# Up projection by seven half-size products for fourteen of twenty-four blocks, on one core

## The reference, cut to what matters

```python
def _moe2_ref(x, w_in, w_out, g_ln):          # x 3072 x 512, w_in 512 x 1024, w_out 1024 x 512
    h = x @ w_in
    e = np.exp(h - np.max(h, axis=-1, keepdims=True))
    solu = h * (e / (np.sum(e, axis=-1, keepdims=True) + 1e-09))
    mu = np.mean(solu, axis=-1, keepdims=True)
    var = np.mean((solu - mu) ** 2, axis=-1, keepdims=True)
    return ((solu - mu) / np.sqrt(var + 1e-06) * g_ln) @ w_out
```

## Time and profile before

| | us |
|---|---|
| three runs: median (lowest, highest) | 971.77 (971.66, 973.21) |
| the profiled execution | 974.78 |
| its span, first to last instruction | 972.9 |
| PE busy | 941.5 (97%) |
| DVE busy | 643.6 (66%) |
| ACT busy | 521.7 (54%) |
| POOL busy | 136.1 (14%) |

### The profile page before, as it was taken

The page is one execution under the profiler, slowest core; times in us unless marked ns, Lnnn a source line. Parts: engine busy times, 40 slices in busy tenths (PEclk is TensorE's granted clock), DMA queues, the critical chain, the costliest instruction groups (busy, mean ns, idle before and its releaser), DMA issues.

```text
span 972.9 us, 14652 instructions
## 1 busy us (share of the span) xinstructions
PE 941.5 (97%) x5334; PEld 832.9 (86%) x5334; DVE 643.6 (66%) x1065; ACT 521.7 (54%) x911; POOL 136.1 (14%) x170
## 2 busy tenths in 40 slices
PE   7979999999999999999999999999999999999996
PEld 4666787787799999999999999999988888888875
DVE  3767885786778755454568877777475775666641
ACT  3554654555555533342546554555477876666632
POOL 4313401101115330000044001010100000000000
PEclk9989999999999999999999999999999999999999
DMA  9746635626153413131374617250520154351533
GB/s 264 215 155 201 183 153 174 184 115 182 55 210 120 157 71 130 49 115 66 111 247 143 229 52 248 87 191 17 170 75 32 27 137 96 88 141 34 112 86 84
DMA packets 103847, 126.61 MB, mean 130 GB/s; under 512 B 8160, under 2 KB 84320, under 8 KB 103776
## 3 DMA queue, kind: packets, MB, share of 16 engines
q1 hardware_dynamic: 98320, 109.28, 36.6%
q0 software_dynamic: 4736, 15.73, 4.7%
q10 hardware_dynamic: 720, 0.66, 0.3%
HBM read 77.41 MB, written 37.75 MB: 118 GB/s over the span
## 4 chain that ended last, share of the span: by engine, by line
PE 79%; DVE 7%; DMA 4%; issue 3%; ACT 3%; SPq 2%; POOL 2%; DVEq 0%; ACTq 0%; POOLq 0%
PE psum L949 10%; PE psum L952 10%; PE psum L951 10%; PE psum L385 8%; PE psum L386 8%; PE psum L387 8%; PE psum L985 6%; PE psum L987 6%; PE psum L988 6%; PE psum L842 3%; PE psum L876 2%; PE psum L866 2%; PE psum L855 2%; DMA w_raw<-weights 1%; DMA v_buf<-v_rows 1%
## 5 line engine op out<-in xcount | busy, mean ns | idle before, releaser
L949 PE MATMUL psum<-xo_hi,w_hi 128*128 128x384 f32 x560 | 195.1, 348 | 7.8 <-DVE psum L1658 2.6
L951 PE MATMUL psum<-xo_lo,w_hi 128*128 128x384 f32 x560 | 188.3, 336 | 0.0
L952 PE MATMUL psum<-xo_hi,w_lo 128*128 128x384 f32 x560 | 188.1, 336 | 0.0
L949 PEld LDWEIGHTS psum<-xo_hi,w_hi 128*128 128x128 f32 x560 | 105.8, 189 | 13.9 <-DVE xo_lo L1644 4.1
L951 PEld LDWEIGHTS psum<-xo_lo,w_hi 128*128 128x128 f32 x560 | 105.9, 189 | 0.8 <-issue 0.3
L952 PEld LDWEIGHTS psum<-xo_hi,w_lo 128*128 128x128 f32 x560 | 105.8, 189 | 0.0
L1163 ACT ACTIVATE xo_hi<-b 128x768 fp32r<-128x768 f32 x84 | 70.6, 846 | 63.2 <-PE psum L988 49.5
L1538 DVE TENSOR_TENSOR xo_lo<-b,xo_hi 128x768 fp32r<-128x768 f32 x84 | 81.2, 969 | 34.5 <-ACT xo_hi L1163 34.3
L385 PE MATMUL psum<-w_out_hi,ln_t_hi 128*128 128x512 f32 x192 | 75.1, 391 | 2.1 <-DVE ln_t_lo L1775 2.1
L1658 DVE TENSOR_TENSOR psum<-psum,p_buf 128x384 f32<-128x384 f32 x48 | 27.1, 564 | 75.0 <-PE psum L952 75.0
L385 PE MATMUL psum<-w_in_hi,x_hi 128*128 128x512 f32 x192 | 75.3, 392 | 0.4 <-ACT h_buf L1284 0.4
(11 more groups left out here) (142 smaller groups left out, 2025.2 us busy)
## 6 DMA issues: line engine op xcount, KB each, us to landing
act_dram<-act_buf SPq DMA_DIRECT2D x48, 384.0 KB, 2.4
b<-act_dram SPq DMA_DIRECT2D x48, 384.0 KB, 4.9
ln_t<-z SPq DMA_DIRECT2D x80, 128.0 KB, 3.1
kq_buf<-k_t SPq DMA_DIRECT2D x32, 192.0 KB, 2.7
kq_buf<-q_t SPq DMA_DIRECT2D x64, 96.0 KB, 3.0
q_dec<-q_t SPq DMA_DIRECT2D x32, 192.0 KB, 2.5
w_raw<-weights POOLq DMA_DIRECT2D x12, 512.0 KB, 4.4
x_dram<-x_tile SPq DMA_DIRECT2D x4, 1536.0 KB, 6.0
```

The costliest lines, as they stand in the source:

```text
L949: pe.matmul(dst, hi[:, cols], xo_hi[:, i, kc, :], start=i in (P1, P7) and kc == 0, stop=False, skip_group_check=True)
L951: pe.matmul(dst, hi[:, cols], xo_lo[:, i, kc, :], start=False, stop=False, skip_group_check=True)
L952: mm = pe.matmul(dst, lo[:, cols], xo_hi[:, i, kc, :], start=False, stop=kc == HK - 1, skip_group_check=True)
```

## The change

The up projection of blocks 10 to 23 is done for seven pairs k of blocks (2 x 128 tokens), as seven products of 128 tokens by 256 features by 512 columns, two rows of three matmuls each. All seven stand on PE ahead of the pair's two down projections.
- The four sums of weight blocks (8 pieces of 128x512) are made by POOL in the second tile of the down stage, stored to `act_dram`, loaded back by POOL in the last stage through two staging buffers, and split by ACT `t_high` and DVE `t_low`. The pieces of P4 take the place of weights that the last plain `up` reads.
- The sums of the activations (`s_raw`) are made for every pair by POOL `make_s`; ACT `s_high` and DVE `s_low` split the seven operands in three parts.
- The results go together in three PSUM banks: ACT `copy_xy` and `copy_p7`, DVE `add_u3` and `add_c22`, ACT `copy_up` for three quarters of h.
- z has one buffer, `squares` serves both squarings, SP loads one pair at a time. SP waits for the weight sums ahead of two loads of the stage before.
- ACT's and DVE's orders are rewritten by pair.

```diff
@@ memory @@
-            z0 = sb(c, "z0", [P, F2C, PARTS, BLOCKS, 32])
-            z1 = sb(c, "z1", [P, F2C, PARTS, BLOCKS, 32])
+            z = sb(c, "z", [P, F2C, PARTS, BLOCKS, 32])
@@ names @@
+        UX, UV, UY = 0, 2, 1
+        UP_ORDER = (P1, P7, P6, P2, P5, P4, P3)
+        FIRST_PAIR = 5
+        T_PIECES = [(p, a) for p in (P7, P6, P5, P4) for a in range(HK)]
@@ SP @@
                     sp.wait_ge(x2_stored[s], DMA * 2)
+                    sp.wait_ge(t_summed, len(T_PIECES))
                     load_x2(0, 0)
             sp.wait_ge(in2_lo_ready, 1)
+            sp.wait_ge(t_summed, len(T_PIECES))
             load_in2(CHUNK_RING)
...
+            def load_up(k):
+                if k > 0:
+                    sp.wait_ge(s_lo_ready, 3 * k)
+                else:
+                    sp.wait_ge(x2_lo_ready, FIRST_PAIR)
+                load_x2(0, 2, k)
...
-                if t + 2 < C_TILES:
-                    load_pair(t + 2)
-                store_out(t - 1, 3)
                 for j in range(3):
+                    if j % 2 == 0 and pair_up(t, j) is not None and pair_up(t, j) + 1 < PAIRS:
+                        load_up(pair_up(t, j) + 1)
+                    if j == 0:
+                        store_out(t - 1, 3)
@@ POOL @@
+            def sum_t(p, a, at):
...
+                    pool.wait_ge(t_summed, at)
+                    pool.wait_ge(t_stored, DMA * at)
+                pool.tensor_tensor(t_sum[:], first, second, ALU.subtract).then_inc(t_summed, 1)
+                pool.wait_ge(t_summed, at + 1)
+                pool.dma_start(t_store(T_PIECES.index((p, a))), t_sum[:]).then_inc(t_stored, DMA)
...
+            def load_t(i):
+                if i > 1:
+                    pool.wait_ge(t_lo_ready, i - 1)
+                pool.dma_start(t_stage(i)[:], t_store(i)).then_inc(t_loaded[i % 2], DMA)
+            def make_s(k):
...
+                pool.wait_ge(x2_loaded[0], DMA * (4 + k))
+                if k > 0:
+                    pool.wait_ge(s_lo_ready, 3 * k)
...
+            for i in range(4):
+                load_t(i)
+            make_s(0)
+            for i in range(4, len(T_PIECES)):
+                load_t(i)
+            for k in range(1, PAIRS):
+                make_s(k)
@@ PE @@
+            def up_product(k, i):
+                if i in (P1, P2):
+                    pe.wait_ge(s_lo_ready, 3 * k + 1)
+                else:
+                    pe.wait_ge(s_lo_ready, 3 * k + 3)
+                if k == 0 and i in (P4, P5, P6, P7):
+                    pe.wait_ge(t_lo_ready, T_PIECES.index((i, HK - 1)) + 1)
+                if i == P1:
+                    at_least(pe, up_c11_copied, k)
+                elif i == P7:
+                    at_least(pe, up_c21_copied, k)
+                elif i in (P6, P2):
+                    pe.wait_ge(up_xy_copied, k + 1)
+                elif i in (P5, P4):
+                    pe.wait_ge(up_u3_ready, k + 1)
+                else:
+                    pe.wait_ge(up_c22_ready, k + 1)
...
                 for j in range(BLOCKS):
-                    if run_up_of(t, j):
-                        both_up(*run_up_of(t, j))
+                    if pair_up(t, j) is not None and j % 2 == 0:
+                        for i in UP_ORDER:
+                            up_product(pair_up(t, j), i)
                     both_down2(t, j)
@@ ACT, a step from tile 1 on @@
+                    if j % 2 == 0:
+                        if j > 0:
+                            scale_out(t, j - 1)
+                        elif t > 1:
+                            scale_out(t - 1, 3)
+                        ln_high(t, j, 0)
+                        copy_xy(k)
+                        ln_high(t, j, 1)
+                        if k == 0:
+                            for i in (4, 5):
+                                t_high(i)
+                        copy_p7(k)
+                        if k == 0:
+                            for i in (6, 7):
+                                t_high(i)
+                        square_solu(*last_of(k))
+                        deviation_of_pair(last_of(k)[0], last_of(k)[1] // 2)
+                        copy_up(k, P2, UX, 0, 0, up_c11_copied)
+                        copy_up(k, P4, UV, 1, 0, up_c21_copied)
+                        copy_up(k, P3, UY, 0, 1, up_c12_copied)
+                        if k + 1 < PAIRS:
+                            s_high(k + 1, 0)
+                        continue
+                    exponent(*a)
                     both_high(t, j)
...
+                    exponent(*b)
+                    scale_out(t, j - 1)
+                    if k + 1 < PAIRS:
+                        s_high(k + 1, 1)
+                        s_high(k + 1, 2)
+                    else:
                         both_high(*next_block(t, j))
...
+                    square_solu(*a)
@@ DVE, turn_blocks and a step from tile 1 on @@
-                        at_least(dve, ln_t_moved[i], DMA * PARTS * (t - 2))
+                        at_least(dve, ln_t_moved[i], DMA * PARTS * (t - 1))
...
+                    if j % 2 == 0:
+                        both_low(t, j)
+                        if k == 0:
+                            for i in (4, 5):
+                                t_low(i)
+                        add_u3(k)
+                        invert_pair(last_of(k)[0], last_of(k)[1] // 2)
+                        add_c22(k)
+                        turn_up(last_of(k)[0], last_of(k)[1] - 1)
+                        turn_up(*last_of(k))
+                        if k == 0:
+                            for i in (6, 7):
+                                t_low(i)
+                        if k + 1 < PAIRS:
+                            s_low(k + 1, 0)
+                        continue
+                    row_max_up(k, 0)
+                    row_max_up(k, 1)
                     both_low(t, j)
...
+                    take_up(*a)
+                    take_up(*b)
+                    if k + 1 < PAIRS:
+                        s_low(k + 1, 1)
+                        s_low(k + 1, 2)
```

More of the change, by code:

```diff
@@ L227, in retention_moe_kernel @@
             squares = sb(c, "squares", [P, F2])
-            x2_hi0 = sb(c, "x2_hi0", [P, KC, 2 * P], F32R)
+            with ExitStack() as pair:
+                x2_hi0 = sb(pair, "x2_hi0", [P, KC, 2 * P], F32R)
+            up_p7 = sb(c, "up_p7", [P, BANK])
+            sb(c, "gap5", [P, 2 * KC * P - BANK])
             h_buf = sb(c, "h_buf", [P, 2, F2])
@@ L1423, in stage_c @@
                     copy_h(2, 0, 0)
-                    x2_high(2, 1)
+                    for part in range(3):
+                        s_high(0, part)
                     copy_h(2, 0, 1)
@@ L1849, in stage_c @@
                     x2_low(1, 1)
+                    for i in (0, 1):
+                        t_low(i)
                     row_max(1, 0)
@@ L1864, in stage_c @@
                     take_up(1, 3)
-                    x2_low(2, 1)
+                    for part in range(3):
+                        s_low(0, part)
                     row_max(2, 0)
@@ L1871, in stage_c @@
                     take_up(2, 0)
+                    for i in (2, 3):
+                        t_low(i)
                     row_max(2, 1)
```

230 lines of the change are left out of this document (189 added, 41 removed).

## The result

The changed kernel takes **1005.5 us** (median of 4 runs, 1001.6 to 1008.8) where the kernel before took 972.1: ratio 1.034 (95% interval 1.031 to 1.037), 33 us slower. The forecast was 992.6, with a range up to 1002. The profiled execution took 1004.3, its span is 1002.5 (972.9 before), the mean granted clock 0.982 (0.993).

A forecast was written before the change was run, and what follows sets the result against it. PE, busy 97% of the span, was taken as the bound. First pair +13.6, ordinary pairs -0.3 each, tile starts +2.0, +2.0, +1.4, end +0.2, clock +1.8, POOL beside DVE +0.8: +20.9 us, 992.6 us; range 984 to 1002.

The forecast's parts named there:

- What goes: Up projections of the seven pairs: 48 matmuls become 42 per pair, 1.36 us each pair, -9.5 us in all.
- Ordinary pair: Pairs away from tile starts: DVE's queue makes the second down 1.05 us late, pair costs 21.45, a gain of 0.3.
- the rival of POOL and normalise: POOL's sums also slow DVE's normalise in ordinary pairs, +2.7 us, giving 995.3 us; chance 0.12.
- First pair: Blocks 10 and 11: late weight pieces and DVE's queue idle PE 11.7 us before P4; +13.6 us for the pair.
- upper bound for the landings: Piece loads of the first pair beside the moves could take longer than 3.7 us, up to +3.6 in the layout.
- Tile starts: Pairs at the start of tiles 2, 3 and 4: late z moves delay P6 and second down; +2.0, +2.0, +1.4 us.
- Clock: Behind the first pair's 11.7 us idle stretch PE runs at half clock for 3.6 us, +1.8; no other wait lowers it.
- Weight sums in the down stage: Eight weight sums on POOL and their stores in the down stage's second tile: cost 0, bounds 0 and 1 us.
- moves land late: Tile starts: z moves land at 4.5 us each and the single buffer costs more, giving 999.3 us; chance 0.12.
- Only the first pair pays: Rival: DVE's chain takes under 8.1 us and moves land in time, +7.2 us, giving 979; chance 0.07.
- faster: Rival: DVE delivers pieces and odd operands in time, PE never waits, gain 9.5 us, giving 962.3; chance 0.05.
- the moves (+6.7): Bound at tile starts: z moves all landing at 4.5 us instead of 3.1 would add 6.7 us.

The follow-up runs named there:

- e3: The changed kernel with the pair's second turn_up behind the odd step's ln_lows and the next low part behind the row_max pair, on DVE; 1000.7 us.
- e7: The changed kernel with the odd step's ln_highs ahead of the first exponent on ACT and its ln_lows ahead of row_max on DVE; 1005.9 us.
- e5: The changed kernel with POOL's four sums of operands cut to 4 of 128 columns from the second pair on; 1004.4 us.
- e1: The changed kernel with unread matmuls in PE's waits: 8 ahead of P6 in first, third, fifth and last pair, 56 ahead of the first pair's P4; 1007.2 us.
- e2: The changed kernel with the first pair's low parts of weight pieces 6 and 7 moved on DVE to right behind add_u3; 997.1 us.
- e4: The changed kernel with the 16 moves of z ahead of the store of block 2 on SP's queue instead of behind it; 991.6 us.
- e6: e2 with two raw buffers of their own for weight pieces 6 and 7, so their loads don't wait for pieces 4 and 5; 994.9 us.
- z_nosum: y_low without the eight weight sums on POOL in the down stage, their stores and their waits; 973.1 us.
- x_mix: The changed kernel with e2, e4 and e6, and e3's order of second turn and low part only in pairs at a tile's start; 978.2 us.
- x_early: The changed kernel with e7, e2, e4 and e6 together; 976.8 us.
- y_low: x_early with the next pair's last two low parts between the two take_ups on DVE and their high parts ahead of scale_out on ACT; 973.2 us.

## Why the prediction was wrong

The direction was right, and so was the chain of the first pair; the size was 12.5 us too small, +33.4 us against the forecast's +20.9. In the profiled executions (29.5 us apart in time) 8.6 of this show; the other 3.9 are where these two executions lie about their medians. By the prediction's own steps:

- **What goes**: right. 42 matmuls went. In a pair without waits the gain is 1.36 us (20.4 for 21.8), as e3 and e7 show.
- **Ordinary pair**, gain 0.3: the chain was right, its size was not. Measured 22.1, 21.6, 22.0, a loss of 0.15 on the mean, so also the sign. The pairs took 1.2 to 1.7 over their 20.4 of matmuls where I had 1.05; POOL's sums are 0.4 of it on the mean (e5), so the rival of POOL and normalise was right in kind and gave 1.1 of its 2.7 us. The chain I named is the one that waited: the orders that take it apart bring 20.4 to 20.9 (e3) and 20.4 to 21.3 (e7).
- **First pair**, +13.6 and +1.8: measured +18.9 (over 22.4 for the steps before, which I had put at 22.0: their wait costs more than the 0.28 in its bracket). The chain was right link by link. P4 starts 24.7 us behind P1 where I had 21.6: pieces 4 and 5 were ready 1.0 later than I had them, 6 and 7 were ready 5.8 us after issue for 4.2, and a normalise beside POOL took 1.13 for 0.81. That is near my upper bound for the landings, 3.6. And 13 matmuls behind P4 ran at half clock where I had 8, 2.6 us for 1.8. The 8 behind P6, which I had excluded ("no such wait in the last stage lowered it"), cost little: P5, which had to wait for its pieces, started 9.3 us behind P1, against 9.1 to 9.2 in e1, e2 and e4, where those 8 ran at full clock. e2 and e6 took P4's wait to 5.4 and 1.3.
- **Tile starts**, +2.0, +2.0 and +1.4: measured +3.9, +4.2 and, in the last, +3.4. **This step failed**, in two terms, the length of the moves and the clock. The start of the moves was right (3.6 us ahead of the pair), their length was not: 13.4 us for 16 directly behind the 256 KB store, where before they started 4 us behind it and took 11.1. ln_high came at 3.7 instead of 2.7, the next x at 15.0 instead of 12.6, and P6 waited 2.1 to 2.2 for 1.2. The odd down waited 2.6 in the third pair, but 1.2 and 1.1 in the fifth and the last, less than the 1.9 I had. Behind P6 of the fifth and the last pair the clock fell too, 1.6 us each, where I had said that waits of this kind in this stage don't lower it. e4 removes P6's wait and the low clock with one line. ACT's two waits in the third pair, which starts at 839.81:

```profile
843.52 0.63 ACT L1475 ACTIVATE ln_t_hi<-ln_t 128x512 fp32r<-128x512 f32 x1 [2.91 <-DMA ln_t<-z]
844.05 0.58 ACT L1533 ACTIVATE psum<-psum 128x512 f32<-128x512 f32 x1
...
854.79 0.63 ACT L1528 ACTIVATE s_hi<-x_raw 128x512 fp32r<-128x512 f32 x1 [2.33 <-DMA x_raw<-x_dram]
```

- **Clock**: 37 half-rate matmuls, about 7.4 us of extra matmul time, in place of 1.8; some of it hid in waits that would have followed (e1).
- **Weight sums in the down stage**, 0: right (z_nosum).
- **Rivals**: "moves land late" came nearest (999.3), with another cause: not each landing, whose median is 3.2 us for the 3.1 of the earlier trace rows, but the rate at which SP issues them behind a store. "Only the first pair pays" and "faster" are what e3 and e4 approach in their pairs, so DVE was never too slow for the pace; its order was.

The range was short for one reason above all. Its upper end, 1002.9, already held the landings (+3.6) and the moves (+6.7) together, but it was cut to 1002, and the clock had a bound downward only (-1.8), where 37 matmuls at half rate instead of 8 took 5.6 us more.

What stays open: why 16 moves take 12.9 us and more right behind a store and 11.1 to 11.8 ahead of it was not tried by itself, nor how much of e4's gain is their length and how much their start, nor what decides whether the clock falls, nor whether the first pair, left in the eight-product form, would let the other six show their 5 us.

## What to carry to other kernels

When a transformation shortens one engine's work, cost the queues that feed it in their order, and above all what stands behind what: here 32 of 33 us came back by another order on the queues of SP, ACT and DVE and by two more staging buffers for POOL's loads, and in the changed kernel's last stage no vector operation beside POOL took more than 0.4 us longer than alone. Cures found one at a time don't add up: the late turn freed DVE and held SP, the early ln_high freed PE to reach a later transfer sooner; after each one look for what now waits for the thing you delayed. And give every new wait of 2 us or more a clock term with a range from nothing to the whole: here the same wait cost 1.6 us or none.

## What the runs showed that I had not expected

- The low clock came behind waits of 2.2 us at P6 in the fifth and last pair (granted clock 0.57 in 892 to 896), not in the third with 2.1, and not in x_mix, x_early and y_low behind 2.2 to 2.3 us at the first pair's P6. In the kernel before no wait of the last stage lowered it. Fourteen profiles have a wait of 2.1 to 2.4 us at the first pair's P6; in six of them half-rate matmuls follow, in eight none, and z_nosum has them where y_low, with the same order in this stage, has not. The same wait may or may not cost 1.6 us; what decides it was not found.
- Matmuls issued into a wait held the clock at 1.00 through 16 us (e1), and the time did not fall.
- The sixteen moves of 128 KB of a later tile start took 11.1 to 11.8 us ahead of a store of 256 KB and 12.9 to 13.8 right behind it (once 14.4, in e1), in each kernel that had one or the other order. In the kernel before, 4 us behind the store, they took 11.1 to 11.6.
